# The second layer's output products of passes 1 and 2 by Strassen's algorithm, in a three-stage transformer kernel on one core

## The reference

```python
out_d = sm_attn(q_d, k_d, v_d)          # coarse attention, 4 x 8 heads, 144 groups of 4 rows
...
x = attention output, as (2304, 512)
x = layer_norm(h * softmax(h)) @ w_out  # h = x @ w_in, 1024 wide
h = x @ w_in                            # second layer: 512 -> 2048
g = h * np.cos(h)
return (g @ w_out).astype(np.float32)   # 2048 -> 512
```

## Time and profile before

| | us |
|---|---|
| median of three runs | 693.91 (693.6 to 694.18) |
| the profiled execution's own time | 693.08 |
| its span, first to last instruction | 691.3 |
| TensorE busy | 679.0 (98%) |
| VectorE, ScalarE, GpSimd busy | 440.2, 407.5, 233.9 |

### The profile page before, as it was taken

How to read it: one execution, slowest core, us unless ns; L and a number is a source line. 1 busy time by engine, 2 the same in 40 slices (tenths; PEclk the granted TensorE clock), 3 DMA queues, 4 the chain that set the end, 5 groups by cost and what they waited for, 6 DMA issues and landing times.

```text
span 691.3 us, 12769 instructions
## 1 busy us (share of the span) xinstructions
PE 679.0 (98%) x4783; PEld 600.2 (87%) x4783; DVE 440.2 (64%) x806; ACT 407.5 (59%) x849; POOL 233.9 (34%) x315
## 2 busy tenths in 40 slices
PE   7999999999999999999999999999999999999998
PEld 4677889889889999999989989889899989898986
DVE  7888964654562324356888888965556676655553
ACT  4669865555564656466666657654445676544444
POOL 6997763553523464501222245600000430000000
PEclk9999999999999999999999999999999999999999
DMA  8962331321100000557544253443222336322202
GB/s 299 321 185 95 117 103 45 110 80 63 38 1 1 1 1 1 183 190 259 191 159 145 108 210 110 157 148 107 107 108 106 123 135 245 123 107 106 107 1 91
DMA packets 18445, 82.77 MB, mean 120 GB/s; under 512 B 1872, under 2 KB 5968, under 8 KB 15056
## 3 DMA queue, kind: packets, MB, share of 16 engines
q1 hardware_dynamic: 18384, 81.96, 33.9%
HBM read 62.56 MB, written 19.40 MB: 119 GB/s over the span
## 4 chain that ended last, share of the span: by engine, by line
PE 94%; DVE 4%; issue 1%; ACT 1%; POOL 1%; POOLq 0%; ACTq 0%
PE ps L1586 28%; PE ps L1563 25%; PE ps L1419 15%; PE ps L1450 15%; PE ps L1434 2%; PE ps L1391 2%; PE ps L1329 1%; PE ps L1377 1%; PE ps L1459 1%; PE ps L1366 1%; PE ps L1351 1%; DVE xT L1123 1%; PE ps L1322 1%; PE ps L1341 1%; DVE turn L1264 1%
## 5 line engine op out<-in xcount | busy, mean ns | idle before, releaser
L1563 PE MATMUL ps<-y_parts,w_parts 128*128 128x384 f32 x1008 | 203.2, 336 | 0.7 <-ACT part L942 0.7
L1563 PEld LDWEIGHTS ps<-y_parts,w_parts 128*128 128x128 f32 x1008 | 180.4, 188 | 15.8 <-ACT part L942 1.1
L1586 PE MATMUL ps<-wo,g_hi 128*128 128x512 f32 x576 | 179.2, 392 | 0.0
L1586 PEld LDWEIGHTS ps<-wo,g_hi 128*128 128x128 f32 x576 | 105.8, 188 | 11.8
L1586 PE MATMUL ps<-wo,g_lo 128*128 128x512 f32 x288 | 114.3, 397 | 0.0
L956 ACT ACTIVATE turn<-h,quarter 128x384 f32<-128x384 f32 x96 | 59.0, 615 | 79.6 <-DVE h L1256 79.3
L1450 PE MATMUL ps<-ln_hi,w_split 128*128 128x384 f32 x384 | 103.2, 339 | 0.0
L1270 DVE TENSOR_TENSOR turn<-h,turn 128x384 f32<-128x384 f32 x96 | 61.7, 643 | 44.0 <-ACT turn L962 44.0
L1256 DVE TENSOR_TENSOR h<-ps,part 128x384 f32<-128x384 f32 x72 | 40.1, 557 | 56.8 <-PE ps L1563 56.6
L1419 PE MATMUL ps<-w_split,x_hi 128*128 128x512 f32 x288 | 73.0, 395 | 0.1
L606 POOL TENSOR_TENSOR y_parts<-xT,y_parts 128x768 fp32r<-128x768 f32 x17 | 32.8, 1947 | 117.5 <-ACT y_parts L831 117.5
(11 more groups left out here) (110 smaller groups left out, 971.1 us busy)
## 6 DMA issues: line engine op xcount, KB each, us to landing
w_parts<-w_kept SPq DMA_DIRECT2D x16, 1792.0 KB, 7.3
w_kept<-w_parts SPq DMA_DIRECT2D x8, 1792.0 KB, 6.7
qk_in<-in_qk SPq DMA_DIRECT2D x16, 586.0 KB, 4.4
vblk<-in_v_blocks SPq DMA_DIRECT2D x16, 384.0 KB, 5.5
v<-in_v_rows SPq DMA_DIRECT2D x16, 288.0 KB
result<-o_sb SPq DMA_DIRECT2D x18, 256.0 KB, 3.8
xT<-in_w_in SPq DMA_DIRECT2D x8, 512.0 KB, 7.8
raw_wo<-in_w_out SPq DMA_DIRECT2D x8, 512.0 KB, 5.9
```

The lines of the kernel that those rows point to most:

```text
L1563: last = nc.tensor.matmul(product_ps(s, k), w[:, m, a, c, :], y_parts[:, n, b, c, :], start=(not adds and c == 0 and m == 0 and n == 0), s ...
L1586: last = nc.tensor.matmul(o_ps(tile), g[n][:, t * P:(t + 1) * P], wo[:, p, w, f, :], start=(first and m == 0), stop=(done and m == 2))
```

## The change: output products by Strassen's algorithm in passes 1 and 2

In pass 0 the output products stay as they were. In passes 1 and 2 they are taken for two halves of the model's columns and the pass's two groups of tokens at once, seven products for eight. The result of these passes has columns of the model as rows (the weights are now the stationary factor, g the moving one), and goes to a second output, which the host's code turns round.

- The weights of these products (`w_out_kept`): three plain quarters A and four sums S for each p, in a high and a low part. In pass 0 GpSimd makes the sums (`make_so`, four operations of 256 columns), ScalarE and VectorE or GpSimd split them (`split_so`), SP stores sums and quarters (`store_so`, `store_a`). There is one buffer for the sums. `split_wo` moves into steps 0 to 7 and waits for the sums of its p. Passes 1 and 2 load 14 blocks of 256 columns for each p (`load_parts`).
- The g side: instead of four splits a step there are seven, in a written list ENTRIES of 14 for each pair of steps, through a ring of six buffers. GpSimd makes the four sums of blocks (`sums`) and the low parts of P6, P7, P4 and P5 (`low`); VectorE makes those of P1, P3 and P2. For the last pair VectorE makes all.
- An entry is two halves of three matmuls of 384 columns. P3 and P2 sum in banks of their own over the pass. P1, P6, P7, P4 and P5 share two banks; behind each, its running total is read out: in the first pair of a pass by ScalarE (a copy), later by VectorE (`add_total`, an addition from PSUM). The next product of the five waits for that reading (`total_read`).
- The first layer's products of passes 1 and 2 stand in pairs now, (P1, P2), (P6, P5), (P7, P3), P4, with two, two, two and one entry behind them (one, two, two, two in odd steps from step 11 on). Steps 8 and 9 have the last 15 units of pass 0 in the entries' place, so that the last pair's 14 entries all stand behind step 23.

```diff
+PART_OF = {P1: (A11, 0), P2: (A12, 3), P6: (S2, 1), P5: (S1, 0), P7: (S3, 2), P3: (S4, 1), P4: (A22, 3)}
+RING = 6
+ENTRIES = []
+for _s in range(JOINS, STEPS - 2, 2):
+    ENTRIES += [(P1, _s), (P1, _s + 1), (P3, _s), (P2, _s), (P6, _s), (P3, _s + 1), (P2, _s + 1), (P6, _s + 1),
+                (P7, _s), (P7, _s + 1), (P4, _s), (P4, _s + 1), (P5, _s), (P5, _s + 1)]
+_s = STEPS - 2
+ENTRIES += [(P3, _s), (P2, _s), (P1, _s), (P1, _s + 1), (P6, _s), (P5, _s), (P3, _s + 1), (P6, _s + 1), (P5, _s + 1),
+            (P7, _s), (P7, _s + 1), (P2, _s + 1), (P4, _s), (P4, _s + 1)]
+ENTRY = {entry: n for n, entry in enumerate(ENTRIES)}
+
+READS = (P1, P6, P7, P4, P5)
+
+
+def by_pool(n):
+
+    p, s = ENTRIES[n]
+    return p in (P6, P7, P4, P5) and s < STEPS - 2
...
+            def store_so(p):
+
+                sp.wait_ge(so_hi_ready, p + 1)
+                sp.dma_start(kept_out[p, :, 0, S1:S1 + 1, :], so_hi[0][:].bitcast(F32)).then_inc(so_hi_stored, DMA)
+                sp.dma_start(kept_out[p, :, 0, S2:S4 + 1, :], so_hi[1][:].bitcast(F32)).then_inc(so_hi_stored, DMA)
+                sp.wait_ge(so_lo_ready, p + 1)
+                sp.dma_start(kept_out[p, :, 1, S1:S4 + 1, :], so_lo.bitcast(F32)).then_inc(so_lo_stored, DMA)
+
+            def store_a(p):
+
+                sp.wait_ge(wo_lo_ready, p + 1)
+                for m in range(2):
+                    sp.dma_start(kept_out[p, :, m, A11:A12 + 1, :],
+                                 wo[:, p, m, :, 0:COLS].bitcast(F32)).then_inc(a_stored, DMA)
+                    sp.dma_start(kept_out[p, :, m, A22, :],
+                                 wo[:, p, m, 1, COLS:2 * COLS].bitcast(F32)).then_inc(a_stored, DMA)
...
+                if p == 2:
+                    store_so(0)
+                    store_a(0)
+                store_so(p - 1)
+                store_a(p - 1)
+            store_so(JOINS - 1)
+            store_a(JOINS - 1)
...
+            def make_so(p):
+
+                pool.wait_ge(wo_loaded[p], DMA)
+                need(pool, so_hi_stored, 2 * DMA * p)
+                need(pool, so_lo_stored, DMA * p)
+                a11, a12 = (raw_wo[:, p, n, 0:COLS] for n in range(2))
+                a21, a22 = (raw_wo[:, p, n, COLS:2 * COLS] for n in range(2))
+                s1, s2, s3, s4 = (so_raw[:, n] for n in range(4))
+                nc.gpsimd.tensor_tensor(s1, a21, a22, ALU.add).then_inc(so_made, 1)
+                nc.gpsimd.tensor_tensor(s3, a11, a21, ALU.subtract).then_inc(so_made, 1)
+                pool.wait_ge(so_made, 4 * p + 1)
+                nc.gpsimd.tensor_tensor(s2, s1, a11, ALU.subtract).then_inc(so_made, 1)
+                pool.wait_ge(so_made, 4 * p + 3)
+                nc.gpsimd.tensor_tensor(s4, a12, s2, ALU.subtract).then_inc(so_made, 1)
+
+            def split_so(p):
+                pool.wait_ge(so_hi_ready, p + 1)
+                for hi, some in ((so_hi[0], slice(0, 1)), (so_hi[1], slice(1, 4))):
+                    last = nc.gpsimd.tensor_tensor(so_lo[:, some], so_raw[:, some], hi[:].bitcast(F32), ALU.subtract)
+                last.then_inc(so_lo_ready, 1)
+
+            def sums(s):
+
+                b11, b22, b12, b21 = acts[s % 4]
+                at = 4 * (s - JOINS)
+                pool.wait_ge(hcos_ready, 4 * s + 3)
+                wait_low(pool, ENTRY[P1, s])
+                nc.gpsimd.tensor_tensor(b11, b12, b11, ALU.subtract).then_inc(t_made, 1)
+                pool.wait_ge(t_made, at + 1)
+                nc.gpsimd.tensor_tensor(b12, b22, b12, ALU.subtract).then_inc(t_made, 1)
+                pool.wait_ge(t_made, at + 2)
+                wait_low(pool, ENTRY[P3, s])
+                nc.gpsimd.tensor_tensor(b22, b22, b11, ALU.subtract).then_inc(t_made, 1)
+                pool.wait_ge(t_made, at + 3)
+                pool.wait_ge(hcos_ready, 4 * s + 4)
+                wait_low(pool, ENTRY[P2, s])
+                nc.gpsimd.tensor_tensor(b21, b21, b22, ALU.subtract).then_inc(t_made, 1)
+
+            def low(p, s):
+                if (p, s) in ENTRY and by_pool(ENTRY[p, s]):
+                    n = ENTRY[p, s]
+                    pool.wait_ge(entry_hi_ready, n + 1)
+                    nc.gpsimd.tensor_tensor(ring_lo[n % RING][:], acts[s % 4][PART_OF[p][1]],
+                                            ring_hi[n % RING][:].bitcast(F32), ALU.subtract).then_inc(pool_lo_ready, 1)
...
-            for s in range(STEPS):
-                q = s // JOINS
-                if q and s % JOINS == 0:
-                    for part in (T3, B22, T4):
-                        split_y(q, part)
+            for s in range(JOINS):
                 if s + 1 < JOINS:
                     for part in (S1, S2, S3, S4):
                         make_w(s + 1, part)
-                if q + 1 < PASSES and s % JOINS == JOINS - 2:
-                    for part in (T1, T3, T2, T4):
-                        make_y(q + 1, part)
-                if q + 1 < PASSES and s % JOINS == JOINS - 1:
-                    for part in (B11, B21, T2, T1):
-                        split_y(q + 1, part)
+                make_so(s)
+                if s < JOINS - 1:
+                    split_so(s)
+                if s == JOINS - 2:
+                    for part in (T1, T2, T3):
+                        make_y(1, part)
+                if s == JOINS - 1:
+                    for part in (B11, B21, T2):
+                        split_y(1, part)
+                    make_y(1, T4)
+                    split_y(1, T1)
...
+            def copy_total(p, s, c):
+
+                act.wait_ge(entry_done, 2 * ENTRY[p, s + 1] + c + 1)
+                if s > JOINS:
+
+                    if p == P5:
+                        act.wait_ge(z_ready, 4)
+                    else:
+                        act.wait_ge(z_stored[READS.index(p)], 2 * DMA)
+                elif p == P1:
+                    act.wait_ge(g_used, 4 * JOINS)
+                else:
+                    for tile in range(6):
+                        act.wait_ge(o_stored[tile], DMA)
+                nc.scalar.activation(totals[p][c][:], z_ps(s, p, c), ACT.Copy).then_inc(total_read[p], 1)
...
                 dve.wait_ge(wo_hi_ready, p + 1)
+
+                dve.wait_ge(so_made, 4 * (p + 1))
...
+            def add_total(p, s, c):
+
+                if s >= JOINS and s % JOINS:
+                    dve.wait_ge(entry_done, 2 * ENTRY[p, s + 1] + c + 1)
+                    dve.wait_ge(total_read[p], reads_of(s - 2, c))
+                    nc.vector.tensor_tensor(totals[p][c][:], z_ps(s, p, c), totals[p][c][:],
+                                            ALU.add).then_inc(total_read[p], 1)
...
+                if s < JOINS:
+                    split_g(s, 0)
+                    split_wo(s)
+                if s == JOINS - 1:
+                    split_so(s)
...
+            def entry(n):
+
+                p, s = ENTRIES[n]
+                first, pair = pair_first(s), (pair_first(s) - JOINS) // 2
+                adds = p in (P6, P7, P4)
+                if p in (P3, P2):
+                    opens, closes = s % JOINS == 0, s % JOINS == JOINS - 1
+                else:
+                    opens, closes = s == first and not adds, s > first
+                if p == P1 or s == STEPS - 2 and p == P3:
+                    pe.wait_ge(parts_loaded[s % 4], DMA * ((s - JOINS) // 4 + 1))
+                wait_low(pe, n)
+                a = PART_OF[p][0]
+                for c in range(2):
+
+                    if p in (P3, P2):
+                        if s == JOINS:
+                            pe.wait_ge(o_copied, 6)
+                        elif s == 2 * JOINS:
+                            pe.wait_ge(z12_steps if p == P3 else z11_ready, c + 1)
+                    elif p == P5 and s == STEPS - 2:
+                        pe.wait_ge(corner_added, 3 * STEPS)
+                        pe.wait_ge(corner_copied, STEPS)
+                    elif s == first and p == P1:
+                        if pair == 0:
+                            pe.wait_ge(o_copied, 2)
+                        else:
+                            pe.wait_ge(total_read[P5], reads_of(s - 2, c))
+                    elif s == first:
+                        pe.wait_ge(total_read[{P6: P1, P7: P6, P4: P7, P5: P4}[p]], reads_of(s, c))
+                    for m, (w, g) in enumerate(((0, ring_hi), (0, ring_lo), (1, ring_hi))):
+                        last = nc.tensor.matmul(z_ps(s, p, c), parts[:, s % 4, w, a, c * P:(c + 1) * P], g[n % RING][:],
+                                                start=(opens and m == 0), stop=(closes and m == 2),
+                                                skip_group_check=adds)
+                    last.then_inc(entry_done, 1)
...
+            for s in range(JOINS + 2, STEPS):
+                for pair, count in zip(((P1, P2), (P6, P5), (P7, P3), (P4,)), (1, 2, 2, 2) if s % 2 else (2, 2, 2, 1)):
+                    for k in pair:
+                        product(s, k)
```

(5 more changed lines are left out.)

550 lines of the change are left out of this document (468 added, 82 removed).

## The result

The changed kernel takes 758.37 us, median of 4 runs (757.61 to 760.75), beside 693.75 us for the kernel before on the same chip (693.05 to 694.18): a ratio of 1.0938, 95% interval 1.0912 to 1.0965. It is slower, as forecast, but by 64.6 us where 9.1 were forecast, far outside the range. The profiled execution has a span of 756.9 us.

What follows compares the result with a forecast made beforehand. TensorE was taken to bound the kernel, busy 679.0 of 691.3 us. Terms -15.6 + 9 + 4 + 3 + 5 + 3.7 = +9.1 us gave 703.0 us; 8 in 10 for 690 to 716, likeliest case 698 to 709.

Steps and rivals of the forecast that it cites:

- step 1: Step 2's first product waits for VectorE, held by GpSimd's sums until the first sums are stored; +9 us (5 to 13).
- steps 6 and 7: Pass 0: VectorE's splits, its losses to GpSimd and later splits of y; +3 us (0 to 8).
- steps 10 to 23: Passes 1 and 2: a pair of steps takes VectorE 30.0 us against TensorE's 29.4; +5 us (0 to 15).
- Matmuls and the end: Matmuls of passes 1 and 2: -15.6 us; behind step 23: +3.7 us (1.5 to 7), from waits and VectorE ending later.
- The half clock behind the wait: After step 1's wait TensorE's clock may fall to half; some us on top, not in the sum.
- Steps 2 to 5: Pass 0: GpSimd's added 5.54 us a step costs VectorE 0.5 a us; +1.0 us a step, +4 (0 to 9).
- later splits of y: GpSimd's splits of y behind its new work, within the +3 us for steps 6 and 7, without a size of their own.
- The third: Rival: the port lock holds for all of GpSimd's time; +32 us without overlap, 712 to 722 with half overlapping; chance 0.2.
- The second: Rival: VectorE's losses fall into its own waits, so the port costs nothing; 691 us, or 684.8; chance 0.2.
- The fourth: Rival: gains and waits cancel within 0.2%, about 1.4 us; chance 0.05.

Runs made afterwards that it cites:

- i1: h2 with GpSimd's sums and low parts of y for pass 1 on 8 columns too, values left out; 696.27 us, beside 695.05 for the kernel before.
- e1: The changed kernel with the stores of p = 0 (sums and A parts) issued ahead of the third store of w_kept in SP's queue; 750.32 us.
- e3: The changed kernel with both moves in SP's queue, that of e1 and that of e2; 737.34 us, ratio 1.0628 to the kernel before.
- e2: The changed kernel with the load for step 8 issued ahead of the last stores of sums and A parts in SP's queue; 747.29 us.
- h3: e3 with GpSimd's sums and low parts of y for pass 1 on 8 columns, values left out; 726.00 us.
- h2: e3 with GpSimd's sums and low parts, and its y work for pass 2 except two y sums, on 8 columns, values left out; 709.18 us.
- h4: e3 with VectorE making all low parts and sums of activations, and GpSimd's y work for pass 2 on 8 columns except two sums; 729.71 us.
- e9: The kernel before with eight unread 320-column scratch additions a step on GpSimd in steps 9 to 13 and 16 to 21; 693.08 us beside 693.72.
- g1: e3 with the splits of output weights' sums in pass 0 made by VectorE at the end of a step, not by GpSimd; 729.94 us.
- e5: e3 with GpSimd's sums and low parts in passes 1 and 2 on 8 columns of 384, values left out; 710.42 us.
- e7: e5 with GpSimd scratch additions of as much time added, which nobody reads or waits for; 719.81 us.

## Why the prediction was wrong

The direction and the engine were right: VectorE, made longer by GpSimd, has no room left, and step 1 has the wait that was named, 9.7 us long and with the clock down. The sum was wrong in two terms above all, steps 6 and 7 and steps 10 to 23.

*Matmuls and the end: right in sum.* In i1, where GpSimd leaves VectorE alone, all from step 8 on takes 253.4 us against 265.9 before: -12.5, where -15.6 + 3.7 = -11.9 was forecast. Behind the last matmul the kernel after needs 7.6 us (749.3 to 756.9) and before 3.3; the +2.5 that I had put on VectorE there was +4.3.

*Step 1: right in its links, 9 became 14.4.* Mis-sized: the issue of the stores (333.8 instead of 326.6). e1 shows the queue's share, 9.9 us. Missing: VectorE's losses beside GpSimd's new split at the start of this step, which hold TensorE for 2.3 us in e1. The half clock behind the wait, named but not in the sum, cost nothing in step 2.

*Steps 2 to 5: 4 became 7.6.* The rate held. In steps 3 to 5 of e3,

```profile
354.53:406.00 51.47, 48.78 (x235) 41.64 (x234) 50.73 (x66) 33.19 (x62) 30.47 (x31) 1.00 0.67 237
```

VectorE has 16.9 us a step against 13.68, GpSimd 10.2 against 3.64: 3.2 lost for 6.5, or 0.50, the rate that I had taken. GpSimd's addition was 6.5 us instead of 5.54 (GpSimd's operations get longer beside VectorE's too). A step is as long as VectorE's work and 0.25 us more, so steps 3 to 5 are 1.5 us longer each, not 1.0. The other 3.2 us are step 2 alone: in e3 it takes 18.87 us with VectorE busy for 18.57 and GpSimd for 12.19.

*Steps 6 and 7: the first failed step, 3 became 23.6.* I had counted VectorE's splits and GpSimd's losses, and not looked at what else stands in SP's queue: the load for step 8, behind seven stores that wait for these very splits (e2: 9.9 us). The "later splits of y" were a remark in that term; with GpSimd's y sums they cost 11.0 us (h3), since operations of 2 us back to back turn 1.2 and 1.3 us of VectorE into 2.9 and 4.5. What h3 leaves is 34.2 us against 31.4: the 2.8 us that were counted.

*Steps 10 to 23: the second failed step.* The forecast had 30.0 us of VectorE for a pair against 29.4, so 0.9 us. In steps 10 to 22 of the kernel after, 13.7 us were lost where the matmuls alone would have won some 14 (h2: 189.8 against 203.9). VectorE's own work was right: 138.7 us in 6.5 pairs are 21.3, I had 21.9. Wrong were three things: GpSimd's y work for pass 2 was in no term (12.1 us of splits, 8.1 of sums); the loss is 0.58 a us, not 0.5, and GpSimd has 22.8 us a pair with the y work, not 16.2; and above all I set VectorE's load against TensorE's as if it could be filled to the last. Steps 18 to 21 of e3, behind all y work, are the case that the forecast had in mind. There VectorE is busy for 57.4 us, 28.7 a pair, less than the 30.0 of the forecast, and still a pair takes 31.6 us where its matmuls take 29.1 and the forecast gave 30.3. h4 shows the same with next to no stops, VectorE being busy for 88% of the 208.1 us.

*The rivals.* The third, "slower still", came nearest in time, but its 712 to 722 is too low too, since no rival held the wait in step 7, and its reason, that VectorE loses all of GpSimd's time, fell: it loses 0.50 to 0.58 of it. The second, "faster: the port costs nothing", fell. That stops cost nothing while VectorE has room is right (e9); the changed kernel has no room. The fourth, no change, fell with it.

Still open: in step 1 why the stores take over 7 us to land (e1), why the real operations stop VectorE more than the scratch additions do, whether another order on VectorE would let h4 go faster, and 11.4 us in steps 1 to 5 (i1) that stay in every run with the output weights' sums whole, of which g1 takes 4.

## What to carry to other kernels

Before an engine is given more work because it is idle half of the time, add up all of its work and its neighbour's in the tightest steps, with what each loses to the other, and expect waits well before the sum reaches the bounding engine's time. Against TensorE's 189.6 us for steps 10 to 22, a VectorE of 138.7 us was covered (h2), one of 147.3 cost 2 us (e5), one of 170.3 cost 11 (e7) and one of 183.9 cost 18 (h4). For every store that is put into an in-order DMA queue, name the next load behind it and the time at which the store's own wait ends. A long wait on a chain should be priced with what it does to the granted clock behind it, but only where TensorE is the limit behind it: 2.6 us in step 8, nothing in step 2.

## What the runs showed of the hardware

- GpSimd's SBUF operations take VectorE's time by an amount that depends on the operations: 0.58 us for each us in steps 10 to 22 (e3 against h2), 0.50 in pass 0, 0.30 for additions of a tile to itself under a VectorE with more room (e9). VectorE's tensor_scalar with one SBUF input is stopped as well (0.35 us alone, up to 2.00), sums that read PSUM aren't: 140 such sums of e3, from the hidden products on, all take 0.54 to 0.56 us. In e3, VectorE and then GpSimd:

```profile
581.02 0.55 DVE L1716 TENSOR_TENSOR total<-ps,total 128x384 f32<-128x384 f32 x1
581.48 1.52 DVE L1673 TENSOR_SCALAR whole<-last_wo 128x384 f32<-128x384 f32 x1
582.92 0.54 DVE L1716 TENSOR_TENSOR total<-ps,total 128x384 f32<-128x384 f32 x1
583.39 1.71 DVE L1679 TENSOR_TENSOR last_wo<-last_wo,whole 128x384 f32<-128x384 f32 x1
...
580.64 4.05 POOL L776 TENSOR_TENSOR y_parts<-xT,y_parts 128x768 fp32r<-128x768 f32 x2
```

- The same three DMA issues on SP (L565, L566, L568) took 1.40, 1.26 and 1.07 us in step 1 and 0.33, 0.43 and 0.37 us in step 7.
- After TensorE had waited 9.7 us, six matmuls took 2.29 us instead of 1.21, so the clock was at 1.2 GHz, not 2.4; the windows of steps 1, 2, 7 and 8 have 0.83 to 0.88. In step 8 this cost 2.6 us (15.46 against 12.88 in h3), in step 2, where VectorE was the limit, nothing.
